# Attention: products with V in plain float32, one head on each half of the TensorE array, result normalised from PSUM

## What is computed

```python
def _attn_ref(q, k, v):                      # (4, 8, 576, 64) each
    ...
    q_rot, k_rot = (rotate(q), rotate(k))
    scores = scale * np.matmul(q_rot, k_rot.transpose(0, 1, 3, 2))
    scores = scores - np.max(scores, axis=-1, keepdims=True)
    attn = np.exp(scores)
    attn = attn / (np.sum(attn, axis=-1, keepdims=True) + 1e-09)
    return np.matmul(attn, v).astype(np.float32)

def reference(**kwargs):
    ...
    attn_out = _attn_ref(**attn_kwargs)
    x = np.ascontiguousarray(attn_out.transpose(0, 2, 1, 3)).reshape(B * S, H * D)
    x = _moe_ref(x=x, **moe_kwargs)
    return _moe2_ref(x=x, **moe2_kwargs)
```

## Time and profile before

| | us |
|---|---|
| median of 3 runs | 1027.17 (1026.3 to 1027.86) |
| profiled execution | 1027.12, its span 1025.3 |
| PE busy | 979.6 (96%) |
| DVE busy | 585.8 (57%) |
| ACT busy | 449.6 (44%) |
| POOL busy | 441.6 (43%) |

### The profile page before, as it was taken

The page is one execution under the profiler, slowest core; times in us unless marked ns, Lnnn a source line. Parts: engine busy times, 40 slices in busy tenths (PEclk is TensorE's granted clock), DMA queues, the critical chain, the costliest instruction groups (busy, mean ns, idle before and its releaser), DMA issues.

```text
span 1025.3 us, 20327 instructions
## 1 busy us (share of the span) xinstructions
PE 979.6 (96%) x6816; PEld 927.7 (90%) x6816; DVE 585.8 (57%) x1143; ACT 449.6 (44%) x1018; POOL 441.6 (43%) x360
## 2 busy tenths in 40 slices
PE   4899999999998999999999999999999999999998
PEld 3898898889888899999999999999999988888886
DVE  3889989998998543343343343343457364444442
ACT  4898999899988511111111111111111243333332
POOL 6778878887873590320320420410467331121200
PEclk9999999999999999999999999999999999999999
DMA  3233223322313101010010010010021000011001
GB/s 91 68 83 84 66 58 92 81 58 68 92 48 97 63 1 61 1 61 0 2 62 0 1 63 0 1 41 0 0 82 41 1 11 21 21 24 27 20 20 42
DMA packets 26979, 42.33 MB, mean 41 GB/s; under 512 B 4928, under 2 KB 15424, under 8 KB 26944
## 3 DMA queue, kind: packets, MB, share of 16 engines
q1 hardware_dynamic: 26944, 41.88, 14.7%
HBM read 28.30 MB, written 4.72 MB: 32 GB/s over the span
## 4 chain that ended last, share of the span: by engine, by line
PE 75%; DVE 10%; issue 6%; POOL 3%; ACT 2%; DMA 2%; DVEq 1%; SPq 1%; ACTq 0%; POOLq 0%
PE ps L1097 29%; PE ps L1131 15%; PE ps L1193 10%; PE ps L1168 8%; PE ps L1078 5%; PE ps L1035 3%; DVE pT_lo L857 3%; PE ps L1062 2%; DVE nmax L848 2%; PE ps L1006 2%; PE ps L1178 1%; ACT pT_hi L722 1%; DVE q_split L899 1%; DVE o_sum L879 1%; DMA kT<-kT 1%
## 5 line engine op out<-in xcount | busy, mean ns | idle before, releaser
L1097 PE MATMUL ps<-x_hi,w_hi 128*128 (+1 forms) x768 | 226.3, 295 | 0.4 <-DVE hid L919 0.4
L1097 PE MATMUL ps<-x_hi,w_lo 128*128 (+1 forms) x768 | 226.1, 294 | 0.0
L1097 PE MATMUL ps<-x_lo,w_hi 128*128 (+1 forms) x768 | 226.0, 294 | 0.0
L919 DVE TENSOR_TENSOR hid<-ps,sig 128x288 f32<-128x288 f32 x96 | 43.9, 458 | 225.7 <-PE ps L1097 213.6
L763 ACT ACTIVATE sig<-ps 128x288 f32<-128x288 f32 x96 | 39.5, 411 | 303.1 <-PE ps L1097 303.1
L1097 PEld LDWEIGHTS ps<-x_hi,w_hi 128*128 128x128 f32 x768 | 144.1, 188 | 0.6 <-DVE hid L919 0.6
L1097 PEld LDWEIGHTS ps<-x_hi,w_lo 128*128 128x128 f32 x768 | 144.1, 188 | 0.0
L1097 PEld LDWEIGHTS ps<-x_lo,w_hi 128*128 128x128 f32 x768 | 144.1, 188 | 0.0
L571 POOL TENSOR_SCALAR w_hi<-raw_w 128x1024 fp32r<-128x1024 f32 x15 | 41.3, 2775 | 225.2 <-PE ps L1131 225.2
L1035 PE MATMUL ps<-kT,qT 128*128 128x288 f32 (+2 forms) x672 | 120.9, 309 | 11.2 <-ACT prob L700 7.9
L848 DVE TENSOR_REDUCE nmax<-ps 128x1 f32<-128x576 f32 x144 | 108.2, 751 | 19.1 <-PE ps L1035 18.3
(11 more groups left out here) (125 smaller groups left out, 2094.2 us busy)
## 6 DMA issues: line engine op xcount, KB each, us to landing
kT<-kT SPq DMA_DIRECT2D x30, 288.0 KB, 4.0
raw_k<-in_k SPq DMA_DIRECT2D x16, 288.0 KB, 2.8
raw_q<-in_q SPq DMA_DIRECT2D x16, 288.0 KB, 2.8
out_y<-y_sb SPq DMA_DIRECT2D x36, 128.0 KB, 2.4
raw_v<-in_v SPq DMA_DIRECT2D x32, 128.0 KB, 2.7
raw_w<-in_moe_w_gate SPq DMA_DIRECT2D x6, 512.0 KB, 3.7
raw_w<-in_moe_w_val SPq DMA_DIRECT2D x6, 512.0 KB, 4.7
raw_w<-in_moe_w_out SPq DMA_DIRECT2D x6, 512.0 KB, 5.8
```

Source lines behind the costliest of these rows:

```text
L1097: last = nc.tensor.matmul(gv_ps[f][n], w, x, start=m == 0, stop=m == len(todo) - 1)
```

## The change

V is no longer cut into pieces: SP loads it straight into one of two buffers `v_sb`. The transposed probabilities are written once, as float32, into one of two buffers `pT` and `pK`; of the eleven transposes ScalarE copies K, KTR, B1 and A3, VectorE the other seven. There are two shares per pair, queries 0 to 255 and 256 to 575, each for both heads: every product is float32 by float32 with 64 columns of weights (V of one head), and the heads take turns, the first into PSUM partitions 0 to 63, the second into 64 to 127. The tails of the keys (64 rows) of the two heads lie on different rows too. A pair takes 20 products of half the array's width in place of 40 of its full width. VectorE then multiplies the PSUM result by the reciprocals twice (`normal`): once into `x_f` and once, rounded, into `x_hi`. `low`, `add`, `NORM`, `VH`, `VL` and `XH` are gone. `XL` now handles the pair of the step before and waits for the second of `normal`'s semaphores `x_norm`.

```diff
-        SHARES = [(0, 0, MAIN // 2), (1, 0, MAIN // 2), (0, MAIN // 2, S), (1, MAIN // 2, S)]
-        OQ = S - MAIN // 2
+        SHARES = [(0, MAIN // 2), (MAIN // 2, S)]
...
-        raw_v = alloc(at, "raw_v", [P, SLOTS, D])
-        v_split = [alloc(at, f"v_split{u}", [P, 2 * MT, 2, D], F32R) for u in range(2)]
-        v_tail = [alloc(at, f"v_tail{u}", [P, 2, 2, D], F32R) for u in range(2)]
+        v_sb = [alloc(at, f"v_sb{u}", [P, SLOTS, D]) for u in range(2)]
...
-        pT_hi = alloc(at, "pT_hi", [P, MT, 2 * S], F32R)
-        pT_lo = alloc(at, "pT_lo", [P, MT, 2 * S], F32R)
-
-        pK_hi = alloc(at, "pK_hi", [P, S], F32R)
-        pK_lo = alloc(at, "pK_lo", [P, S], F32R)
+        pT = [alloc(at, f"pT{u}", [P, MT, 2 * S]) for u in range(2)]
+        pK = [alloc(at, f"pK{u}", [P, S]) for u in range(2)]
...
-        ORDER_POOL = ["RQ", "RK", "XL", "QL", "VL", "KL", "NORM"]
-        AHEAD = {"B3": -1, "K": -1, "TQ": -1, "KTR": -1, "R": -1, "PV": -1, "INV": -1, "XH": -2, "XL": -2, "NORM": -1,
...
+        ORDER_POOL = ["RQ", "RK", "XL", "QL", "KL"]
+        AHEAD = {"B3": -1, "K": -1, "TQ": -1, "KTR": -1, "R": -1, "PV": -1, "INV": -1, "XL": -1,
...
             def load_v(p):
 
-                if not early(p, 1):
-                    sp.wait_ge(v_ready, num(p) * 4)
+                if not early(p, 2):
+                    sp.wait_ge(pv_done, num(p) * 2 - 2)
                 heads = v.rearrange("b h (p t) d -> p (b h) (t d)", t=SLOTS)
+                dst = v_sb[par(p)]
...
                                             ALU.subtract).then_inc(k_ready, 1)
-                elif name == "VL":
-                    pool.wait_ge(v_hi, num(p) * 4 + 4)
-                    for n, (raw, hi, lo) in enumerate(v_parts(p)):
-                        if n >= 2:
-                            pool.wait_ge(v_ready, num(p) * 4 + n)
-                        nc.gpsimd.tensor_tensor(lo, raw, hi.bitcast(F32), ALU.subtract).then_inc(v_ready, 1)
-                    pool.wait_ge(v_ready, num(p) * 4 + 4)
-                    if step == PAIRS - 1:
-                        lows(0, 0)
                 elif name == "XL":
-                    hold(x_hi_ready, num(p) + 1)
+                    hold(x_norm[1], num(p) + 1)
                     cols = bass.ds(num(p) * S, S)
                     nc.gpsimd.tensor_tensor(x_lo[:, cols], x_f[:], x_hi[:, cols].bitcast(F32),
                                             ALU.subtract).then_inc(x_ready, 1)
-                elif name == "NORM":
-                    bank, before = use("R", step)
-                    pool.wait_ge(tr_out[bank], before + 1)
-                    pool.wait_ge(o_read, num(p) * 4 + 4)
-                    if not early(p, 1):
-                        pool.wait_ge(x_ready, num(p))
-                    nc.gpsimd.tensor_tensor(x_f[:], o_sum[:], rrep[:], ALU.mult).then_inc(x_norm, 1)
+                if step == PAIRS - 1 and name == "XL":
+                    lows(0, 0)
 
...
-            def hi(name, p, step):
+            def turned(name, p, step):
...
-                if not early(p, 1):
-                    shares = {"A0": 1, "A1": 1, "B0": 2, "B1": 2, "A2": 3, "A3": 3}.get(name, 4)
-                    act.wait_ge(pv_done, num(p) * 4 - (4 - shares))
-                for dst, part in p_parts(name, src, pT_hi, pK_hi):
+                for dst, part in p_parts(name, src, par(p)):
                     last = nc.scalar.activation(dst, part, ACT.Copy)
-                last.then_inc(p_hi, 1)
-
-            def low(n, p):
-
-                act.wait_ge(pv_done, num(p) * 4 + n + 1)
-                h, a, b = SHARES[n]
-                r0, r1 = h * D, (1 - h) * D
-                nc.scalar.activation(o_low[r0:r0 + D, 0:b - a], o_ps[r1:r1 + D, 0:b - a], ACT.Copy
-                                     ).then_inc(low_ready, 1)
+                last.then_inc(tr_out[bank], 1)
 
             def first_piece(name, p):
...
-            def lo(name, p, step):
+            def turned(name, p, step):
 
                 bank, before = use(name, step)
-                dve.wait_ge(p_hi, splits_before(name, step) + 1)
-                places = zip(p_parts(name, tr_ps[bank], pT_lo, pK_lo), p_parts(name, tr_ps[bank], pT_hi, pK_hi))
-                for (dst, part), (had, _) in places:
-                    last = nc.vector.tensor_tensor(dst, part, had.bitcast(F32), ALU.subtract)
+                dve.wait_ge(tr_full[bank], before + 1)
+                for dst, part in p_parts(name, tr_ps[bank], par(p)):
+                    last = nc.vector.tensor_copy(dst, part)
                 last.then_inc(tr_out[bank], 1)
...
+            def normal(n, p, step):
+
+                a, b = SHARES[n]
+                bank, before = use("R", step)
+                dve.wait_ge(pv_done, num(p) * 2 + n + 1)
+                dve.wait_ge(tr_out[bank], before + 1)
+                if n == 0 and not early(p, 1):
+                    dve.wait_ge(x_ready, num(p))
+                nc.vector.tensor_tensor(x_f[:, a:b], o_ps[:, 0:b - a], rrep[:, a:b], ALU.mult).then_inc(x_full, 1)
+                cols = bass.ds(num(p) * S + a, b - a)
+                nc.vector.tensor_tensor(x_hi[:, cols], o_ps[:, 0:b - a], rrep[:, a:b], ALU.mult).then_inc(x_norm[n], 1)
...
             def pv(n, p, step):
 
-                bank, before = use("K" if n < 2 else "KTR", step)
+                bank, before = use("K" if n == 0 else "KTR", step)
                 pe.wait_ge(tr_out[bank], before + 1)
                 if n == 0:
-                    pe.wait_ge(tails_clear, 5)
-                    pe.wait_ge(v_ready, num(p) * 4 + 4)
-                if not (early(p, 1) and n == 0):
-                    pe.wait_ge(o_read, num(p) * 4 + n)
-                vs, (h, a, b) = v_split[par(p)], SHARES[n]
-                todo = [(vs[:, h * MT + t, :, :], x[:, t, h * S + a:h * S + b]) for t in range(MT) for x in (pT_hi, pT_lo)]
-                todo += [(v_tail[par(p)][:, h, :, :], x[:, a:b]) for x in (pK_hi, pK_lo)]
-                for m, (w, x) in enumerate(todo):
-                    last = nc.tensor.matmul(o_ps[:, 0:b - a], w.rearrange("p c d -> p (c d)"), x, start=m == 0,
-                                            stop=m == len(todo) - 1)
+                    pe.wait_ge(v_in, num(p) * 48 + 48)
+                    if not early(p, 1):
+                        pe.wait_ge(x_norm[1], num(p))
+                else:
+                    pe.wait_ge(x_norm[0], num(p) + 1)
+                vs, pt, pk, (a, b) = v_sb[par(p)], pT[par(p)], pK[par(p)], SHARES[n]
+                rows = [slice(h * TAIL, (h + 1) * TAIL) for h in range(2)]
+                todo = [(vs[:, h * MT + t, :], pt[:, t, h * S + a:h * S + b], h) for t in range(MT) for h in range(2)]
+                todo += [(vs[rows[h], 2 * MT, :], pk[rows[h], a:b], h) for h in range(2)]
+                for m, (w, x, h) in enumerate(todo):
+                    last = nc.tensor.matmul(o_ps[rows[h], 0:b - a], w, x, start=m < 2, stop=m >= len(todo) - 2)
                 last.then_inc(pv_done, 1)
...
-            BETWEEN = {"TQ": (0, 1), "PV1": (2,), "PV2": (3,)}
+            BETWEEN = {"TQ": (0, 1), "PV0": (2,), "R": (3,)}
```

More of the change, by code:

```diff
@@ L199, in build @@
         pv_done = sem("pv_done")
[L200 to L203, removed]
+        x_norm = [sem(f"x_norm{n}") for n in range(2)]
+        x_full = sem("x_full")
         x_ready = sem("x_ready")
@@ L384, in cos_twice @@
             return cos_sb[:].unsqueeze(2).broadcast_to([P, SLOTS, 2, HALF])
-        def v_parts(p):
-            vs, tails = v_split[par(p)], v_tail[par(p)]
-            heads = [(raw_v[:, h * MT:(h + 1) * MT, :], vs[:, h * MT:(h + 1) * MT, h, :],
-                      vs[:, h * MT:(h + 1) * MT, 1 - h, :]) for h in range(2)]
-            for h in range(2):
-                rows = slice(h * TAIL, (h + 1) * TAIL)
-                heads.append((raw_v[rows, 2 * MT, :], tails[rows, h, h, :], tails[rows, h, 1 - h, :]))
-            return heads
         block = ctx.enter_context(nc.Block())
@@ L708, in hi @@
                 if name in ("R", "KTR") and not early(p, 1):
-                    act.wait_ge(x_norm, num(p))
+                    act.wait_ge(x_norm[1], num(p))
                 if name == "R":
@@ L743, in item @@
             def item(name, p, step):
-                if name[:2] == "PV":
-                    low(int(name[2]), p)
-                elif name == "KH":
+                if name == "KH":
                     first_piece(name, p)
@@ L749, in item @@
                     exps(int(name[1:]), p)
-                elif name in SPLIT or name == "R":
-                    hi(name, p, step)
+                elif name in TURNED or name == "R":
+                    turned(name, p, step)
                 else:
                     qk_out(name, p, step)
-                if step == PAIRS and name == "TQ":
+                if step == PAIRS and name == "K":
                     sigmoid(0, 0)
-                if step == PAIRS and name == "PV0":
```

(30 more changed lines are left out.)

38 lines of the change are left out of this document (14 added, 24 removed).

## The result

The changed kernel takes **1109.9 us** (median of 4 runs, 1103.5 to 1110.7) where the kernel before, run beside it, takes 1027.5: a ratio of 1.079, 95% interval 1.075 to 1.083. The forecast was 1080, slower, with 1027 to 1125 as its range. The profiled execution took 1110.65 us, 83.5 more than the profiled one of before; the forecast had 52.5 more. The sign, the place and the mechanism were right, 31 of the 83.5 us were missing. One of the four runs took 1103.5 us, at a mean granted clock of 0.975 where the others had 0.966, so a difference of a few us against this kernel is uncertain.

What follows compares the result with a forecast made beforehand. No engine alone set the step before; afterwards a closed loop through GpSimd's queue does: 4.35 + 5.8 + 3.45 + 5.4 + P (5.3) = 24.3 us against 20.2, 14 times + 57.4, less 4.9, giving 1080 us, range 1027 to 1125.

Steps and rivals of the forecast that it cites:

- The queue decides: GpSimd's QL stands behind XL, which waits for PV1; T starts 4.35 us after PV1's stream, TensorE stands 3.75.
- From T to S0, 5.8: Last key block to next pair's first score tile: fixed 5.8 us by copy and DMA swap, TensorE standing 1.8.
- P = 5.3: TensorE's time per step for V's products: plain float32 with two heads on two halves costs 5.3 us, as before.
- Drains: Upper case for V's products on TensorE: P = 6.3 with drains, a step of 25.6 us, 1098 us in all.
- S0 to the end of S2, 3.45: TensorE's stretch over the first score tiles of a step: 3.45 us, including 0.55 of waiting.
- A0 to S5, 5.4, including 0.35 of waiting at k1: TensorE's stretch of the step from A0 to S5: 5.4 us, with k1 waiting 0.35 behind B0's copy.
- The slower clock: Rival: gaps on TensorE slow the work between T and S0 to 8 us from 5.8; + 31, 1111 us; chance 0.12.
- The sum: Attention's step becomes 24.3 us against 20.2, 14 times + 57.4, less 4.9 at the ends: + 52.5, 1080 us.
- Cheap float32: Rival for V's products: one pass; P = 1.3 in pairs, 1016 us, chance 0.04; P = 2.6, 1036 us, 0.05.
- no overlap: Rival: the two heads' products on the array's halves do not overlap; P = 10.6, 1164 us; chance 0.10.
- half overlap: Rival: only a product's last pass runs beside the next head's first; P = 8, 1123 us; chance 0.07.
- the loop doesn't close: Rival: GpSimd's QL does not stall T; step 20.5 us, 1027 us within 8; chance 0.07.

Runs made afterwards that it cites:

- experiment 1: The changed kernel with GpSimd's XL moved behind QL and KL: 1050.3 us, ratio 1.024.
- experiment 4: The changed kernel with 24 useless float32r products on TensorE ahead of T, to fill its stand: 1101.7 us, ratio 1.073.
- experiment 3: The changed kernel with all of a share's products of head 0 ahead of those of head 1, instead of taking turns: 1191.5 us (one run).
- Experiment 5: The changed kernel with VectorE's copy of B0 ahead of the two multiplications after PV0: 1102.6 us, ratio 1.074.
- order_alone: The kernel before with its own products and one wait added, GpSimd's XL held until share PV2 of this step's pair: 1089.2 us, ratio 1.060.
- pv1_late: The changed kernel with XL behind QL and KL, and PV1 behind q0 on TensorE and behind A2 on VectorE: 1043.1 us, ratio 1.016.
- tuned1: pv1_late with B0's copy ahead of the multiplications after PV0, and ScalarE's copy of R ahead of S2's exponential: 1037.3 us, ratio 1.010.
- tuned2: tuned1 with S2's exponential ahead of the copies of KTR and R on ScalarE: 1033.2 us, ratio 1.005.

## Why the prediction was right, and where it was short

*The queue decides.* Right, and shown from both sides: the wait alone in the kernel before costs 62 us, taking it out of the changed kernel gives back 60. The link from the end of PV1's stream to T was forecast at 4.35 us and is 4.19 (159.16 to 163.35); TensorE stands 3.38 us where 3.75 was forecast. That 60 and 62 are so near is chance: in the kernel before PV3 still fills the swap and the stand is 2.8 us, and both numbers hold a part of the slower pace.

*From T to S0, 5.8.* S0 is the last four products of a row of fourteen. In the step shown the row behind the fourteen starts at 169.81, so S0, 0.53 before it, at 169.28, which is 5.93 after T. In the next step T starts at 189.00 and S0, counted in the same way, at 195.66, 6.66 after T: there the slower clock stretches the work beyond the swap. At full clock the 5.8 holds well (5.62 in experiment 1, 5.68 in 4); TensorE's work in it was set too low, as it stands 1.15 and 1.14 us, not 1.8.

*P = 5.3.* Measured 2.46 + 2.99 = 5.45. The estimate by piece products, four on half the columns and two heads at once, came within 0.15. In experiment 3 one head's five products of 256 columns take 2.44 us, 0.49 each, where a float32r product of as many columns takes 0.118 (1.18 for ten): 4.1 times as long. How a float32 product is made inside TensorE no run shows; the four were my estimate, and 4.1 is what was measured. The row I called the nearest, the float32 transpose at 0.74 ns per column, was not: the products take 1.9. It gave 4.3, and I kept 5.3 for the other reason.

*Drains.* The 1098 us of the forecast has P = 6.3, a microsecond a step more for drains, and no run shows a drain. What the runs show in its place: a share of 256 columns in which the heads take turns is 2.46 us, and one head's half of it by itself 2.44 (experiment 3). Four times five float32r products at 0.118 us would be 2.36 (an estimate); a share is 0.1 us above it, and P, at 5.45, is 0.15 above the 5.3 that has no drains in it.

*S0 to the end of S2, 3.45.* It is 3.70 (169.28 to 172.98).

*A0 to S5, 5.4, including 0.35 of waiting at k1.* **This term failed most**: 6.37. The work was costed, but not that VectorE's multiplication needs ScalarE's copy of R, which runs behind KTR's four small copies and an exponential. That copy stood there before as well; new is that VectorE waits for it, where GpSimd's NORM did. VectorE waits 0.63, B0's copy stands behind it, k1 waits 0.64. I had counted that two multiplications stand ahead of B0's copy and not whom they wait for. Experiment 5 removes the wait and 0.63 of the stretch. Of the other 0.34 of the 0.97, 0.29 lie between k0 and S4 (177.60 to 178.37 in the step shown, where such a row takes 0.48, 152.65 to 153.13 before); the profile has S4's weight load waiting 0.26 us for an exponential there.

*The slower clock.* I made it a rival of its own, + 31 us at 0.12. It was an addition to the forecast, not another case: it is there right after T in 13 of 14 steps, and costs about 8 us (experiment 4), not 31, because much of TensorE's work after the stand lies beside the swap of kT anyway. That this rival's 1111 us is the measured time is luck: its price for the clock was four times too high, and it left out the 0.97 above. I priced all of the stretch from T to S0 at twice its 4 us; the slow pace ends 3.7 us after T in the step shown and 5.3 in the next, and 1.14 us of what it adds falls into the wait for the swap. What the rows show of it are four transposes in 0.73 us instead of 0.38, at a granted clock of 0.51.

*The sum.* The mean step of 13 is 26.26 us (end of PV1's stream at 53.53, 79.10 ... 394.96), 1.96 above the 24.3 forecast. In the step shown, the links make + 1.34: - 0.16, + 0.13, + 0.25, + 0.97 and + 0.15. The remaining 0.62 is what the slow pace adds in other steps, in the mean. Over 14 steps that is 18.8 + 8.7 = 27.4, and with the 52.5 forecast 79.9 of 83.5. The last 3.6 lie at the start and the end of attention, where I had 4.9 coming back. S0 of pair 1 starts at 37.95, 0.4 later than before and not half a microsecond earlier. From S0 of pair 15 to the row behind the last share are 34.5 us (405.1 to 439.66), where I had 31.8 and the kernel before took 36.2.

*The rivals that fell.* Cheap float32 (P of 1.3 or 2.6) fell by P itself, no overlap and half overlap likewise. Experiment 3 shows how near "no overlap" was: with the two loops in another order it is true. That the loop doesn't close fell by T's 3.4 us, 12 times in 12.

*And the estimates of the experiments* were mostly too low: order_alone left out the clock, pv1_late and tuned1 took a removed wait at its whole length (22 and 12 us too low). In tuned2 TensorE's own work is 12.6 + 5.45 = 18.05 us and the step 20.58: 2.5 us of waiting, as in the kernel before (2.3). VectorE is busy 68% and ScalarE 64% there, against 91% before, and the waiting is still there. My reading, which no experiment shows by itself, is that it is made less by load than by the ways through four engines: scores, maximum, exponential, transposes.

So what does the change bring by itself? With an order that suits it, + 0.5% (tuned2), with the order that it came with, + 7.9%. It takes nothing off TensorE, which has work for 18 of the 20.6 us of a step, since the products with V cost it as much in the new form as in the old (5.45 against 5.3 us). That a still better order makes the new form faster isn't excluded; none of the three tried did.

## What to carry to other kernels

When a step of a slow side engine is moved to a later input, look at what stands behind it in that engine's queue and who waits for that, not at the step itself: here the place of one name in GpSimd's order decided 60 of 83 us. Work taken off engines that don't set the step gave no time back here, though it was about a quarter of VectorE's and ScalarE's (14.0 and 13.1 us busy a step, from 18.4 and 18.3). And cost a wait by whom it waits for, also for instructions that only changed places: the term missed here was a multiplication that waited for another engine's copy.

## What the runs showed of the hardware

- A plain float32 product of 256 columns, on 64 columns of weights, took 0.49 us (five in 2.44, 165.16 to 167.60 in experiment 3), a float32r product of 256 columns, on 128 columns of weights, 0.118 us (ten in 1.18): 4.1 times as long. Ten float32 products show as twenty records in the profile (x16 and x4).
- Two heads on two 64-column halves took 2.46 us together when products of the two alternated (172.98 to 175.44 in the changed kernel), where one took 2.44; with one head's products in a row the two took 4.88 (experiment 3).
- With a stand of 3.4 us in each step of 26 the granted clock was 0.83 from 185 to 205 us; with the stand filled by useless products it was 1.00 from 145 to 165 and as the mean of the run, and the median was 8 us less (1101.7 to 1109.9). The clock records in the changed kernel's trace have 1.00 and 0.50: 14 stretches at 0.50, of 3.4 or 6.8 us each, between 57.7 and 402.5. They are 75 us together, which fits the mean of 0.966 over 1108.8 us. Some 37 us of work at most could be lost in them (an estimate, half of the 75), and 8 were paid. The rest would have fallen into waits.
- In the first 25 us of the program four transposes took 0.71 us start to start (23.63 to 24.34) where they take 0.38 later, though the profile shows a granted clock of 1.00. The 1.00 says nothing there: the clock records begin 26.2 us into the span in the trace of before and 27.0 in that of after, and the windows ahead of them read 1.00 all the same. After a stand in the steady steps four transposes took 0.73 us, and there the granted clock shows 0.51.
